# Zero products in TensorE's two first waits, and a level loop rotated by one group

## The chip, the cores and the metric

The kernel runs on one core of a Trainium2 chip. The metric is device time in microseconds (us) for one execution, as the median of several runs.

## The reference

Three stages follow one another for 4 batches of 768 tokens. First a gated linear attention with 8 heads of 48 columns, whose state is decayed and updated at every token:

```
for t in range(S):
    state = alpha[:, :, t, :, None] * state + np.einsum('bhd,bhe->bhde', k[:, :, t], v[:, :, t])
    y[:, :, t] = np.einsum('bhd,bhde->bhe', q[:, :, t], state)
```

Then a block with a low-rank mix over the tokens and a ReLU network of width 1536:

```
h = x.transpose(0, 2, 1) @ U @ V
u = x + h.transpose(0, 2, 1)
x = u + np.maximum(u @ w_ch1, 0.0) @ w_ch2
```

Then a second gated network: a product with `w_in` and a ReLU, a normalised half that is mixed over the tokens by `w_spatial`, a gate and a product with `w_out`. Inputs and output are float32.

## The kernel before

Five engines run programs of their own and meet only at semaphores. TensorE (PE) does all matrix products, VectorE (DVE), ScalarE (ACT) and GpSimd (POOL) the work between them, and SyncE (SP) issues the loads.

The attention of one batch is cut into two groups of four heads. In the text group 0 is the one whose tiles are `K`, `Q`, `AL`, `Qd`, `Ad` and `A`, and group 1 of the first batch the one whose tiles end in `_side`. Within chunks of 128 tokens the scores are built over eight levels, n = 0 to 7: level n pairs blocks of `block_size(n)` tokens. For each of the levels 0 to 5 and each group g the same round is made:

- ACT spreads the queries of the level into `Qd` (`first_spread`, L1080; two copies). It needs PE's products of the level before, since `Qd` is one buffer, and the queries scaled by POOL (`scale_q`, L670).
- PE multiplies them with the keys (`first_level`, which calls `square_scores`, L778): 48 small products of 32 by 32, which the trace records as 96. For group 0 they go to `SB`, for group 1 to `ZB`.
- DVE takes the scores under a mask (`take`, L1397) into `Ad` and scales the keys for the next level (`scale_k`, L1377).

PE's code for this is a hardware loop of six turns over n, with group 0 and group 1 in the turn. Levels 6 and 7 follow in straight code (L826 and L838), then transposed keys (L853), key-value products (L866), outputs (L883, L892) and the token mix (L916). After that PE runs the dense products of the first network (L901, L989 to L991), with the attention of the next batch in between.

At the very start nothing but loads and memsets can run. SP issues queries, decays and keys of group 0 and then of group 1. DVE clears four areas (L1678, L1679, semaphore `zeroed_s`), waits for the decays, and multiplies them up in `first_decay` and `totals` (L1384). PE waits for `zeroed_s`, for the keys (`ld_k`) and for the first spread queries. ACT later copies totals of group 1 into the bank `ZB0` (`total_copies`, L1117).

`w2h` holds weights of the first network, which are loaded and split long after the start. `ZB0` is the first of three banks of PSUM that group 1 and the network share.

Of the kernel before, what the change touches and what calls it, by code (L numbers as in the profile page):

```python
# [7 lines left out]
F32 = mybir.dt.float32  # L8
# [5 lines left out]
P = 128  # L14
# [14 lines left out]
GROUPS = HEADS // (2 * PAIRS)  # L29
# [15 lines left out]
MASKED = 6  # L45
# [141 lines left out]
def vector_slots(slots):  # L187

    out, waiting = [], []
    for j, unit in enumerate(UNITS1):  # L190
        now = []
        for g, n in slots[j]:
            now += waiting
            waiting = [(g, n, piece) for piece in range(vector_pieces(n))]
            now += waiting
            waiting = []
            if n == START_STEP:
                now.append((g, START, 0))
            if n == PREFIX_STEP:
                now.append((g, PREFIX, 0))  # L200
        if not slots[j]:
            now += waiting[:1]
            waiting = waiting[1:]
        out.append(now)
    assert not waiting
    return out


def vector_pieces(n):

    return 2 if n < MASKED else NKV if n == KV_STEP else int(n < LEVELS)
# [14 lines left out]
SPLIT_V = {(0, T_STEP): [0], (1, T_STEP): [1], (1, KV_STEP): [2]}  # L226
IN_PSUM = (3, 4, 5, 2)
SPLITS2 = {2: W1_PIECES + 3, 3: W1_PIECES + 4, 4: W1_PIECES + 5}
VECTOR_SLOTS = [vector_slots(slots) for slots in SLOTS]


def build(nc, q, k, al, v, u_w, v_w, w1, w2, win, wst, wout, bias, ident_d, mask_d, out):
# [3 lines left out]
    with ExitStack() as ctx:  # L236
# [11 lines left out]
        def sem(name):  # L248
            return ctx.enter_context(nc.semaphore(name))
# [6 lines left out]
        V_in, _ = place("V_in", [RANK3, SEQ], o)  # L256
# [13 lines left out]
        early, _ = place("early", [P, STAGE * PIECE], o + 2 * 4 * DB * FF1 + 4 * STAGE * PIECE)  # L270
# [4 lines left out]
        w2h, o = place("w2h", [P, F1B, DM], o, F32R)  # L275
# [54 lines left out]
        x2, _ = place("x2", [P, DB, SEQ], at_xn)  # L330
        x2l, _ = place("x2l", [P, DB, SEQ], at_xn, F32R)
# [5 lines left out]
        winf, _ = place("winf", [P, DB, FF2], o)  # L337
        winl, o = place("winl", [P, DB, FF2], o, F32R)
        BF, _ = place("BF", [P, 7, HS, TH], o)
# [9 lines left out]
        AF, _ = place("AF", [P, 7, HS, HF], o)  # L349
        AL, o = place("AL2", [P, 7, HS, HF], o, F32R)  # L350
        gf, _ = place("gf", [P, FGB, SEQ], o)
        gl, o = place("gl", [P, FGB, SEQ], o, F32R)
        partial, _ = place("partial", [P, FGB, SEQ], o)
# [4 lines left out]
        wof, _ = place("wof", [P, FGB, DM], o)  # L358
# [14 lines left out]
        ZB = [ps(f"ZB{i}") for i in range(DB)]  # L373
# [77 lines left out]
        gl_done = sem("gl_done")  # L451

        passed = sem("passed")
        stored = [sem(f"stored{i}") for i in range(2)]


# [200 lines left out]
        def _(pool):  # L657
# [88 lines left out]
            for b in range(BATCH - 1):  # L746
                for g in range(GROUPS):
                    for n in range(2, LEVELS):
                        scale_q(b + 1, g, n)
                        if b == g == 0 and n - 1 in SPLITS2:  # L750
                            split_low(SPLITS2[n - 1])
                        if g == 0 and b:
# [20 lines left out]
        def _(pe):  # L773
# [9 lines left out]
            def first_level(g, n):  # L783

                w = space(0, g)
                pe.wait_ge(ld_k[g], 16)
                pe.wait_ge(qd_ready[g], 2 * n + 2)

                pe.wait_ge(k_ready[g], n + 1)
                square_scores(level_bank(w, n, True), w.K, w.Qd[0]).then_inc(score_done[g], 1)  # L790
# [185 lines left out]
            def down(b, f):  # L976
# [5 lines left out]
                for d in range(DB):  # L982
# [7 lines left out]
                    nc.tensor.matmul(bank, w2l[:, i, cols], hi, start=False, stop=False)  # L990
                    nc.tensor.matmul(bank, w2h[:, i, cols], lo, start=False, stop=(i == F1B - 1)).then_inc(z_done, 1)  # L991

            def two_group(b, j, first):
                stage, i, h, _, _, at = TWO.groups[j]
                bank = TB[at]
                th = slice(h * TH, (h + 1) * TH)
                last_use, wrapped = TWO.last_use(j)
                if not wrapped:
                    read(pe, TWO, last_use, b)
                elif not first:  # L1000

                    read(pe, TWO, last_use, b - 1)
                else:

                    pe.wait_ge(h_lo, NF * BATCH)
                    if bank in ZB:
                        pe.wait_ge(z_read, NU * (BATCH - 1) + NU - DB + ZB.index(bank) + 1)
                if stage == "v":
                    pe.wait_ge(win_lo, DB)

                    pe.wait_ge(x2_lo, DB * (b + 1))
                    last = split_product(bank[:, 0:FG],
                                         lambda x, d: (x2h, x2l)[x][:, d, i * P:(i + 1) * P],
                                         lambda y, d: (winh, winl)[y][:, d, FG:FF2], [(d, d) for d in range(DB)], DB)
                elif stage == "g":
                    last = split_product(bank[:, 0:TH],
                                         lambda x, d: (winh, winl)[x][:, d, i * P:(i + 1) * P],
                                         lambda y, d: (x2h, x2l)[y][:, d, th], [(d, d) for d in range(DB)], DB)
                elif stage == "s":
                    k = SEVEN.index(i)  # L1020
                    fp = slice(h * P, (h + 1) * P)
                    pe.wait_ge(b_lo, SPLIT_B.index(k) + 1)
                    pe.wait_ge(ah_done, 7 * b + k + 1)
                    for m in range(HS):
                        for y, w in enumerate((BH[k][:, m, :], BL[:, k, m, :])):
                            nc.tensor.matmul(bank[:, 0:TH], AH[:, k, m, fp], w, start=(i in OPENS and m == y == 0),  # L1026
                                             stop=False, skip_group_check=True)
                    pe.wait_ge(al_done, 7 * b + k + 1)
                    for m in range(HS):
                        last = nc.tensor.matmul(bank[:, 0:TH], AL[:, k, m, fp], BH[k][:, m, :],  # L1030
                                                start=False, stop=(m == HS - 1), skip_group_check=True)
                else:
                    pe.wait_ge(wo_lo, 1)
                    rows = slice(i * P, (i + 1) * P)
                    gates = NHALF * FGB * b + (NHALF * FGB if i < HS else 3 * FP)
                    pe.wait_ge(gh_done, gates)
                    for f in range(FGB):
                        for w in (woh, wol):
                            nc.tensor.matmul(bank[:, 0:DM], gh[:, f, rows], w[:, f, :], start=(f == 0 and w is woh),  # L1039
                                             stop=False, skip_group_check=True)  # L1040

                    pe.wait_ge(gl_done, gates)
                    for f in range(FGB):
                        last = nc.tensor.matmul(bank[:, 0:DM], gl[:, f, rows], woh[:, f, :], start=False,
                                                stop=(f == FGB - 1), skip_group_check=True)
                last.then_inc(two_done, 1)

            pe.wait_ge(zeroed_s, 4)
            with pe.Fori(0, MASKED) as n:
                for g in range(GROUPS):  # L1050
                    first_level(g, n)
            for g, n in LAST_STEPS:
                att_step(0, g, n, True)

# [13 lines left out]
            for j in range(TWO.n):  # L1068
                two_group(0, j, True)
# [5 lines left out]
        def _(act):  # L1075
# [35 lines left out]
            def total_copies(g):  # L1111
                w = space(0, g)

                act.wait_ge(tot_ready[g], 4)
                act.wait_ge(zeroed_s, 4)
                for L in (4, 8, 16):
                    nc.scalar.copy(psum_total(w, L), w.tot[L]).then_inc(tot_psum[g], 1)  # L1117

# [196 lines left out]
            for b in range(BATCH - 1):  # L1315
                for j, (kind, i, _) in enumerate(UNITS1):
                    for g, n in SLOTS[b][j]:
                        att_step(b + 1, g, n, False)
                        if b == g == 0 and n in SPLITS2:
                            split_high(SPLITS2[n])  # L1320
                        na, ng = after(b + 1, g)
# [38 lines left out]
        def _(dve):  # L1360
# [83 lines left out]
            def first_level(g):  # L1444

                w = space(0, g)
                dve.wait_ge(ld_mask, 16)
                dve.wait_ge(zeroed_s, 4)
                take(0, g, 0)
                scale_k(0, g, 0)  # L1450
                dve.wait_ge(qd_ready[g], 4)
                dve.wait_ge(tot_ready[g], 1)
                qq = odd(Q[g][:, :], 1).rearrange("p n l -> p (n l)")
                nc.vector.tensor_tensor(qq, qq, w.tot[2], ALU.mult).then_inc(q_ready[g], 1)
# [217 lines left out]
            def aggregate(b, i):  # L1672
                dve.wait_ge(stat_done, NT * b + i + 1)
                dve.sem_inc(passed, 1)
                nc.vector.bn_aggr(mv[:, i, :], stats[:, i, :]).then_inc(mv_done, 1)

            for w in (main_space, side_space):
                nc.vector.memset(w.Ad[:, :, :, :], 0.0).then_inc(zeroed_s, 1)  # L1678
                nc.vector.memset(w.KVB[:, UNITS * BLOCK:512], 0.0).then_inc(zeroed_s, 1)  # L1679
# [32 lines left out]
            for b in range(BATCH):  # L1712
                for j, (kind, i, _) in enumerate(UNITS1):
                    if b < BATCH - 1:
                        for g, n, piece in VECTOR_SLOTS[b][j]:
                            na, ng = after(b + 1, g)
# [60 lines left out]
```

## Time and profile before

| | us |
|---|---|
| median of 3 runs | 728.19 |
| lowest and highest run | 728.19, 728.77 |
| span of the profiled execution, first to last instruction | 723.9 |
| PE busy in that span | 697.6 (96%) |
| DVE, ACT, POOL busy | 394.7, 340.2, 213.5 |

Of the profiled execution the trace gives only the span; the runs are timed around it, so some 4.3 us (728.19 - 723.9) lie outside the span. A busy PE is not a PE at full rate: at its slower clock the same products fill more time.

### The profile page before, as it was taken

How to read it: one execution, taken by the hardware profiler on the slowest of the kernel's cores; microseconds unless marked ns; L12 is line 12 of the kernel's file. 1: busy time of each engine (PE TensorE's matmuls, PEld its weight loads, DVE VectorE, ACT ScalarE, POOL GpSimd, SP SyncE). 2: the span in 40 equal slices, each digit the busy share in tenths (PEclk: the TensorE clock that was granted, in tenths of full speed). 3: DMA queues.
4: the chain of work that ended last, by engine and by line, in shares of the span. 5: the costliest groups of instructions: out<-in, count | busy, mean ns of one | idle time of the engine just before them, and what ended most of it. 6: DMA issues, size and time to landing. Idle time of an engine off the chain costs nothing.

```text
span 723.9 us, 25699 instructions
## 1 busy us (share of the span) xinstructions
PE 697.6 (96%) x11336; PEld 661.9 (91%) x11336; DVE 394.7 (55%) x666; ACT 340.2 (47%) x575; POOL 213.5 (29%) x143
## 2 busy tenths in 40 slices
PE   2799999999999999999999999999999999999998
PEld 2688989899899999999999999999998998999998
DVE  6898766546645644755552415125834842871671
ACT  5987655463654454555453332335523432532422
POOL 6704660410540310350220331461360060043022
PEclk9999999999999999999999999999999999999999
DMA  8415410411301221401100341011110101101001
GB/s 359 170 48 182 150 46 4 152 49 37 122 11 39 86 79 39 156 3 47 36 3 3 116 139 64 32 44 56 65 45 23 66 23 43 65 0 65 0 0 65
DMA packets 16524, 49.48 MB, mean 68 GB/s; under 512 B 1616, under 2 KB 9552, under 8 KB 15920
## 3 DMA queue, kind: packets, MB, share of 16 engines
q1 hardware_dynamic: 16432, 48.09, 19.1%
q8 instruction: 77, 1.26, 0.7%
q14 instruction: 15, 0.12, 0.1%
HBM read 38.65 MB, written 9.44 MB: 66 GB/s over the span
## 4 chain that ended last, share of the span: by engine, by line
PE 90%; DVE 3%; ACT 1%; issue 1%; DVEq 0%
PE HB L901 25%; PE ZB L989 7%; PE ZB L991 7%; PE ZB L990 7%; PE SB L901 6%; PE SB L1026 5%; PE SB L778 4%; PE ZB L901 4%; PE SB L883 2%; PE SB L1030 2%; PE ZB L1039 2%; PE ZB L1026 2%; PE SB L892 2%; PE SB L1039 2%; PE SB L838 1%; DVE K L1377 1%
## 5 line engine op out<-in xcount | busy, mean ns | idle before, releaser
L1557 DVE SCALAR_TENSOR_TENSOR hid_lo<-HB,hid_hi 128x384 fp32r<-128x384 f32 x92 | 51.2, 557 | 138.3 <-ACT hid_hi L1233 137.8
L1233 ACT ACTIVATE hid_hi<-HB 128x384 fp32r<-128x384 f32 x92 | 45.3, 492 | 157.6 <-PE HB L901 157.4
L989 PE MATMUL ZB<-hid_hi,w2h 128*128 128x384 f32 x288 | 98.2, 341 | 0.0
L901 PE MATMUL HB<-uh,w1h 128*128 128x384 f32 x276 | 97.7, 354 | 0.2 <-DVE ul L1553 0.2
L991 PE MATMUL ZB<-hid_lo,w2h 128*128 128x384 f32 x288 | 96.5, 335 | 0.0
L990 PE MATMUL ZB<-hid_hi,w2l 128*128 128x384 f32 x288 | 96.3, 334 | 0.0
L901 PE MATMUL HB<-uh,w1l 128*128 128x384 f32 x276 | 92.5, 335 | 0.2 <-issue 0.2
L901 PE MATMUL HB<-ul,w1h 128*128 128x384 f32 x276 | 92.5, 335 | 0.0
L1080 ACT COPY Qd<-Q 48x768 f32<-48x768 f32 x84 | 73.2, 871 | 14.2 <-POOL Q L670 5.2
L727 POOL TENSOR_TENSOR gl<-gf,gh 128x384 fp32r<-128x384 f32 x32 | 33.6, 1048 | 144.1 <-ACT gh L1273 143.8
L670 POOL TENSOR_TENSOR Q<-Q,bk 112x768 f32<-112x768 f32 x14 | 25.5, 1824 | 162.9 <-ACT Qd L1080 162.9
L778 PEld LDWEIGHTS SB<-Qd,K 112*32 112x32 f32 x4032 | 42.0, 116 | 22.6 <-issue 17.2
L670 POOL TENSOR_TENSOR Q<-Q,small 112x768 f32<-112x768 f32 x26 | 42.7, 1641 | 65.3 <-PE SB L826 31.2
L778 PE MATMUL SB<-Qd,K 112*32 112x32 f32 x4032 | 46.7, 205 | 13.3 <-DMA K<-in_k 9.3
L1377 DVE TENSOR_TENSOR K<-K,small 112x768 f32<-112x768 f32 x26 | 48.8, 1877 | 16.8 <-PE SB L838 9.5
L989 PEld LDWEIGHTS ZB<-hid_hi,w2h 128*128 128x128 f32 x288 | 54.0, 188 | 0.9
L1649 DVE BATCH_NORM_STATS2 stats<-vf 128x6 f32<-128x512 f32 x24 | 16.5, 692 | 69.8 <-ACT vf L1277 69.8
L901 PEld LDWEIGHTS HB<-uh,w1h 128*128 128x128 f32 x276 | 51.7, 187 | 2.9 <-DVE ul L1553 0.3
L990 PEld LDWEIGHTS ZB<-hid_hi,w2l 128*128 128x128 f32 x288 | 54.1, 188 | 0.0
L991 PEld LDWEIGHTS ZB<-hid_lo,w2h 128*128 128x128 f32 x288 | 54.1, 188 | 0.0
L901 PEld LDWEIGHTS HB<-uh,w1l 128*128 128x128 f32 x276 | 51.9, 188 | 0.5 <-issue 0.5
L901 PEld LDWEIGHTS HB<-ul,w1h 128*128 128x128 f32 x276 | 51.8, 188 | 0.0
(269 smaller groups left out, 1519.4 us busy)
## 6 DMA issues: line engine op xcount, KB each, us to landing
Q<-in_q SPq DMA_DIRECT2D x8, 768.0 KB, 5.8
AL<-in_al SPq DMA_DIRECT2D x7, 768.0 KB, 4.6
K<-in_k SPq DMA_DIRECT2D x7, 768.0 KB, 4.4
Vt<-in_v SPq DMA_DIRECT2D x8, 576.0 KB, 3.8
mid<-x2s SPq DMA_DIRECT2D x8, 576.0 KB, 3.5
x<-mid SPq DMA_DIRECT2D x4, 1152.0 KB, 5.2
out<-o_sb SPq DMA_DIRECT2D x24, 192.0 KB, 1.8
x2s<-in_w SPq DMA_DIRECT2D x9, 384.0 KB, 4.3
```

The costliest lines, as they stand in the source:

```text
L670: nc.gpsimd.tensor_tensor(qq, qq, t.broadcast_to([ROWS, FLAT // (2 * L), L]), ALU.mult).then_inc(q_ready[g], 1)
L727: nc.gpsimd.tensor_tensor(gl[:, f, t], gf[:, f, t], gh[:, f, t].bitcast(F32), ALU.subtract).then_inc(gl_done, 1)
L778: last = nc.tensor.matmul(bank[j * BLOCK:(j + 1) * BLOCK, u * BLOCK:(u + 1) * BLOCK], keys[:, first_key:first_key + BLOCK], queries[:, u, ...
L901: last = nc.tensor.matmul(dst, weights(x, w), moving(y, m), start=(n == 0 and x == y == 0), stop=(n == total - 1 and y == 1))
L989: nc.tensor.matmul(bank, w2h[:, i, cols], hi, start=(i == 0), stop=False)
L990: nc.tensor.matmul(bank, w2l[:, i, cols], hi, start=False, stop=False)
L991: nc.tensor.matmul(bank, w2h[:, i, cols], lo, start=False, stop=(i == F1B - 1)).then_inc(z_done, 1)
L1026: nc.tensor.matmul(bank[:, 0:TH], AH[:, k, m, fp], w, start=(i in OPENS and m == y == 0), stop=False, skip_group_check=True)
L1080: nc.scalar.copy(space(a, g).Qd[0 if first else n % 2][r, :, hh, :].rearrange("p u (n l) -> p u n l", l=block_size(n)), targets(Q[g][r, :] ...
L1233: nc.scalar.activation(hid_hi[:, i % HID, :], up_bank(i)[:, 0:TILE], ACT.Relu).then_inc(h_hi, 1)
L1377: nc.vector.tensor_tensor(kk, kk, t.broadcast_to([ROWS, FLAT // (2 * L), L]), ALU.mult).then_inc(k_ready[g], 1)
L1557: nc.vector.scalar_tensor_tensor(hid_lo[:, i % HID, :], up_bank(i)[:, 0:TILE], 0.0, hid_hi[:, i % HID, :].bitcast(F32), ALU.max, ALU.subtr ...
```

## The change

DVE clears three rows of `w2h` (128 partitions by 1152 elements) as its first work and raises `spare_zeroed`. PE waits for that, runs 20 products of 128 by 512 on the zeroes into `ZB0`, then level 0 of group 0, then 14 more of these products, and raises `spare_done`. The loop over the levels is turned by one group: group 0's level 0 stands ahead of it, each of five turns runs group 1 of one level and group 0 of the next, and group 1's level 5 stands behind it. ACT waits for `spare_done` before it copies group 1's totals into `ZB0`. The wait of PE for `zeroed_s` comes behind the first 20 products.

```diff
+SPARE_FRONT, SPARE_BETWEEN = 20, 14
...
+            def spare_products(n):
+
+                for _ in range(n):
+                    last = nc.tensor.matmul(ZB[0][:, :], w2h[:, 0, 0:P], w2h[:, 1:3, 0:256], start=True, stop=True)
+                return last
+
...
+            pe.wait_ge(spare_zeroed, 1)
+            spare_products(SPARE_FRONT)
             pe.wait_ge(zeroed_s, 4)
-            with pe.Fori(0, MASKED) as n:
-                for g in range(GROUPS):
-                    first_level(g, n)
+            first_level(0, 0)
+            spare_products(SPARE_BETWEEN).then_inc(spare_done, 1)
+            with pe.Fori(1, MASKED) as n:
+                first_level(1, n - 1)
+                first_level(0, n)
+            first_level(1, MASKED - 1)
...
                 act.wait_ge(zeroed_s, 4)
+                if g:
+                    act.wait_ge(spare_done, 1)
...
+            nc.vector.memset(w2h[:, 0:3, :].bitcast(F32), 0.0).then_inc(spare_zeroed, 1)
             for w in (main_space, side_space):
```

On PE, at the start of the program, these rows stood before (`SB` and `Qd_76` are group 0, `ZB` and `Qd_side` group 1; the branches and register rows are the loop's):

```order
L1049 UNCONDITIONAL_BRANCH
L787 ISA
L789 REGISTER_ALU
L778 MATMUL SB<-Qd_76,K 32x32 x48
L787 ISA
L789 REGISTER_ALU
L778 MATMUL ZB<-Qd_side,K_side 32x32 x48
L1049 REGISTER_ALU
L1049 COMPARE_AND_BRANCH
L826 MATMUL SB<-Q_69,K 32x32 x48
```

and these stand there now:

```order
L999 MATMUL ZB<-w2h 128x512 x20
L781 MATMUL SB<-Qd_76,K 32x32 x48
L999 MATMUL ZB<-w2h 128x512 x14
L1062 UNCONDITIONAL_BRANCH
L790 ISA
L781 MATMUL ZB<-Qd_side,K_side 32x32 x48
L790 ISA
L792 REGISTER_ALU
L781 MATMUL SB<-Qd_76,K 32x32 x48
L1062 REGISTER_ALU
L1062 COMPARE_AND_BRANCH
L781 MATMUL ZB<-Qd_side,K_side 32x32 x48
```

The two blocks of zero products are new; the sequence of the real products, group 0 and group 1 in turn, is the one of before, and the loop's branch has moved from behind group 1 to behind group 0.

On DVE, from the start of its program, before:

```order
L1678 MEMSET Ad 128x768
L1679 MEMSET SB 128x128
L1678 MEMSET Ad_side 128x768
L1679 MEMSET HB 128x128
L1384 TENSOR_TENSOR bk<-AL 112x768
```

and now:

```order
L1693 MEMSET w2h 128x1152
L1695 MEMSET Ad 128x768
L1696 MEMSET SB 128x128
L1695 MEMSET Ad_side 128x768
L1696 MEMSET HB 128x128
L1400 TENSOR_TENSOR bk<-AL 112x768
```

One memset stands ahead of the four others and of the first product of decays; nothing else on DVE has moved.

## Rows read from the trace of the kernel before

**Rows 1.** The page: busy time, granted clock in 40 slices, the chain by engine
```profile
PE 697.6 (96%) x11336; PEld 661.9 (91%) x11336; DVE 394.7 (55%) x666; ACT 340.2 (47%) x575; POOL 213.5 (29%) x143
...
PEclk9999999999999999999999999999999999999999
...
PE 90%; DVE 3%; ACT 1%; issue 1%; DVEq 0%
```

**Rows 2.** Timeline, 0 to 17 us: start, length, engine, line, operation, tiles, idle before
```profile
0.98 0.70 DVE L1678 MEMSET Ad<- 128x768 f32 x1 [0.98 <-PEq L1770]
...
9.28 1.51 PE L778 MATMUL SB<-Qd,K 112*32 112x32 f32 x96 [9.28 <-DMA K<-in_k]
10.12 0.63 DVE L1384 TENSOR_TENSOR small<-small 112x48 f32<-112x48 f32 x3
...
15.00 1.51 PE L778 MATMUL ZB<-Qd_side,K_side 112*32 112x32 f32 x96 [4.21 <-DMA K_side<-in_k]
...
16.12 0.48 ACT L1117 COPY ZB<-bk_side 112x384 f32<-112x384 f32 x1 [0.72 <-DVE small_side L1384]
```

**Rows 3.** Timeline of PE, 36 to 100 us: the same kinds of products early and late
```profile
36.42 1.50 PE L826 MATMUL SB<-Q,K 48*32 48x32 f32 x96 [0.34 <-DVE K L1377]
...
40.33 2.82 PE L838 MATMUL SB<-Q,K 48*64 48x64 f32 x48
...
67.49 1.03 PE L778 MATMUL SB<-Qd,K 112*32 112x32 f32 x96
...
93.26 1.04 PE L826 MATMUL SB<-Q,K 48*32 48x32 f32 x96 [0.59 <-issue]
...
97.78 1.61 PE L838 MATMUL SB<-Q,K 48*64 48x64 f32 x48
```

**Rows 4.** Stretches: from:to length, PE busy, weight loads, DVE, ACT, POOL, clock, DMA
```profile
16.90:25.00 8.10, 5.99 (x384) 5.46 (x384) 6.99 (x11) 7.86 (x11) 3.55 (x2) 1.00 1.04 377
25.00:36.00 11.00, 8.98 (x576) 8.27 (x576) 9.68 (x13) 9.55 (x12) 9.61 (x7) 1.00 0.12 49
36.40:39.65 3.25, 2.49 (x155) 2.32 (x155) 2.96 (x4) 2.12 (x5) 0.00 (x0) 1.00 0.02 5
39.65:44.60 4.95, 4.95 (x119) 4.89 (x120) 4.21 (x7) 4.79 (x10) 0.00 (x0) 1.00 0.02 5
44.60:48.20 3.60, 3.24 (x42) 2.82 (x39) 3.48 (x7) 3.49 (x8) 0.00 (x0) 1.00 0.02 5
```

**Rows 5.** Groups by shape, PE, 44.75 to 45.7 us: the end of L838
```profile
L838 PE MATMUL ZB<-Q,K_side 48*64 48x64 f32 x19 | 1.1, 291 | 0.0
```

**Rows 6.** What DVE waited for, 7 to 49 us: total, times, longest
```profile
DVE bk L1384 <- DMA AL<-in_al: 4.2, 1, 4.2
DVE Ad L1397 <- PE SB L778: 0.8, 2, 0.4
DVE K_side L1377 <- PE ZB L826: 0.7, 1, 0.7
```

**Rows 7.** Timeline of DVE, 7 to 49 us
```profile
11.07 1.01 DVE L1397 COPY_PREDICATED Ad<-masks,SB 128x384 f32<-128x384 uint32 x1 [0.32 <-PE SB L778]
...
21.76 1.05 DVE L1397 COPY_PREDICATED Ad_side<-masks,ZB 128x384 f32<-128x384 uint32 x1 [0.29 <-DVEq L1491]
23.26 1.06 DVE L1397 COPY_PREDICATED Ad<-masks,SB 128x384 f32<-128x384 uint32 x1 [0.45 <-PE SB L778]
...
37.03 0.95 DVE L1377 TENSOR_TENSOR K_side<-K_side,ZB 112x768 f32<-112x768 f32 x1 [0.19 <-DVE Ad_side L1397]
38.08 0.96 DVE L1377 TENSOR_TENSOR K<-K,small 112x768 f32<-112x768 f32 x1
38.95 0.95 DVE L1433 TENSOR_TENSOR Q<-Q,small 112x768 f32<-112x768 f32 x1
40.56 0.96 DVE L1377 TENSOR_TENSOR K_side<-K_side,small_side 112x768 f32<-112x768 f32 x1 [0.65 <-PE ZB L826]
...
46.62 1.45 DVE L1460 COPY bk<-SB 128x448 f32<-128x448 f32 x3
```

**Rows 8.** The chain that ended last, 30 to 70 us
```profile
39.06 0.58 issue
...
48.21 1.10 PE SB L866 x40
```

**Rows 9.** Timeline of ACT, 9 to 50 us
```profile
29.24 1.69 ACT L1080 COPY Qd_side<-Q 48x768 f32<-48x768 f32 x2 [0.30 <-PE ZB L778]
...
48.40 0.37 ACT L1186 COPY bk_side<-ZB 128x224 f32<-128x224 f32 x1
```

**Rows 10.** Timeline of PE, second network: products of 128 by 512
```profile
487.10 0.39 PE L901 MATMUL SB<-winh,x2h 128*128 128x512 f32 x1
487.33 0.39 PE L901 MATMUL SB<-winh,x2l 128*128 128x512 f32 x1
```

More of the change, by code:

```diff
@@ L453, in build @@
         passed = sem("passed")
+        spare_zeroed = sem("spare_zeroed")
+        spare_done = sem("spare_done")
         stored = [sem(f"stored{i}") for i in range(2)]
```

## The prediction

> **What bounds the kernel now.** The page gives PE 96% of the span and 90% of the chain that ended last [rows 1]. So a gain has to come from a place where PE is slow, or where something holds PE up. The change touches only the first 36 us, so I read the timeline there. PE's first products wait for the keys of group 0 until 9.28 us, and group 1's for theirs until 15.00 [rows 2]. Both are waits for a load. Nothing in the change moves a load, so zero products cannot shorten them; they can only change the state in which PE leaves them.
>
> That state shows when one kind of product is compared early and late. The 96 records of L778 take 1.51 us at 9.28 and at 15.00 [rows 2], and 1.03 us at 67.49; L826 takes 1.50 at 36.42 and 1.04 at 93.26; L838 takes 2.82 at 40.33 and 1.61 at 97.78, which is 1.75 times [rows 3]. So PE ran at the lower of its two clocks (1.2 and 2.4 GHz) from the start. In the last products of L838 the mean record is down from 311 to 291 ns [rows 5], so the rise lies near 45 us. The column of the granted clock says full speed all along [rows 1, 4]; where it and the durations disagree I go by the durations. Before the rise PE was busy 5.99 of 8.10 us, 8.98 of 11.00, 2.49 of 3.25, and then 4.95 of 4.95 us [rows 4].
>
> Next: who sets the pace between 9 and 48 us? DVE does. Its waits there are few: 4.2 us for the decays, which end at 7.1, then 0.8 us in two waits for PE's L778 and 0.7 us for L826 [rows 6]. Everything else on it is work, or the short pause of about 0.19 us between `take` and `scale_k` [rows 7]. At 48.21 PE waits for DVE's last copy of transposed keys and is on the chain from there [rows 8]. So what DVE gains by 48 us the kernel gains, and hardly more.
>
> **The change, step by step.**
>
> *The memset.* 768 columns take 0.70 us [rows 2], so 1152 take 1.05, from 0.98 to 2.03. The four others end 1.05 later, at 4.0, and DVE has nothing to do until 7.1 [rows 6]. Cost nothing; without the 4.2 us of waiting for `AL` it would be 1.05.
>
> *The 20 products ahead.* Dense products of 128 by 512 follow each other every 0.227 us at the full clock (487.10 to 487.33) [rows 10]; 23 such steps in a row, from 486.65 to 491.86, have this mean. At the lower clock no row shows them; the nearest bound is L838's 1.75 times, 0.40 us, and the other bound is the ratio of the two clocks, 0.45. I take 0.43. They start at about 2.2. If the clock rises 5 us later, after as much unbroken work as the 4.95 us of rows 4, it is 7.2; 11.6 products are done, and 8.4 more at 0.227 end at 9.1. That is just ahead of the keys at 9.28, so nothing is lost. If the clock rises only at the end, the block ends at 2.2 + 20 x 0.43 = 10.8.
>
> *Level 0 of group 0* then takes 1.03 in place of 1.51 and ends at 10.31. DVE is done with its totals at 10.75 [rows 2] and can go on at once instead of at 11.07: **-0.29 us**, the wait of 0.32 less a start-up of some 0.03.
>
> *The 14 products between* end at 10.31 + 14 x 0.227 = 13.5, before the keys of group 1 at 15.00. At the lower clock they would take 14 x 0.43 = 6.0. ACT's new wait for them is covered, since it copies into `ZB0` only at 16.12 [rows 2]: 2.6 us of cover. Behind it on ACT stand all further spreads, so past 15.8 each microsecond would delay the levels.
>
> *Levels 1 to 5.* Each group of products is 0.48 shorter. DVE waited for one of them: 0.45 at 23.26. The pause between two takes that its own semaphores force is 0.29, as at 21.76 [rows 7], so only **-0.16 us** comes out. In the levels 3 to 5 DVE never waits for PE, and a PE that is earlier only waits longer. ACT gains its 0.30 at 29.24 [rows 9], which DVE doesn't see.
>
> *Level 6.* DVE finishes `K_side` (from 37.03, so at 37.98) 0.45 earlier, at 37.53. It need not wait for L826 of group 0 (36.0 to 37.0 now) and goes on at 37.63 instead of 38.08. `K` and `Q` take 0.87 and 0.95, until 39.45. L826 of group 1 starts at 37.65 and needs 1.04, and perhaps the 0.58 of issue that stands in its middle [rows 8], so it ends by 39.3. `K_side` starts at 39.45 instead of 40.56: the wait of 0.65 is gone, **-0.66 us**. From there DVE is busy without a pause to its copies of the transposes at 46.62 [rows 7]. L838 at 1.61 needs DVE's queries of 40.3 at the latest and is no obstacle.
>
> *The side path on ACT.* Its copies of `bk_side` end at 48.77 (48.40 + 0.37) [rows 9]; ACT gets about 0.9 of it by an earlier L826, so it ends near 47.9, while L866 of group 1 would start at 48.0. It fits with nothing to spare.
>
> *The loop.* The order of the products is kept, and the branch stands where PE has waited for group 1's queries or keys anyway: nothing.
>
> Sum: 0.29 + 0.16 + 0.66 = 1.1 us. Against the profiled execution that is a span of 723.9 - 1.1 = 722.8; with the 4.3 us outside the span, 727.1, against the median of 728.19. The most that DVE's waits for PE can give is 0.8 + 0.7 = 1.5.
>
> **The rivals.**
>
> *The clock falls again in the levels.* In rows 4 PE was busy 82% between 25 and 36 us and the clock stayed low. With products of 1.03 for 1.51 the same stretch is filled to 56%. No row shows the higher clock kept or lost over such a stretch. If it falls before 23 us, only the first 0.29 remains, and the rise at 45 us stays as it was: 727.9. The Trainium skill, "TensorE: Matmul & The Clock Gate", section "A second HAM failure mode: psum-queue depth-cycling", tells of a kernel in which small pauses of PE between groups of products made the clock swing between its two rates; by that rule this case would be the one to expect, and no run here shows it yet.
>
> *The zero products overrun (slower).* The place is the front block. If the clock rises only at its end, level 0 of group 0 starts at 10.8, ends at 11.8 at the full clock, and DVE's take starts about 1.0 later than the 11.07 of before. Of that the later 0.82 comes back: 728.4. If it doesn't rise until the second block has run, level 0 ends at 12.3, the 14 end at 18.3, and group 1's level 0 at 19.8, where it ended at 16.5 before (15.00 + 1.51): +3.3, 731.5, or 730.7 with what comes back. It decides at a front block that ends after 9.7 us, and at a second one that ends after 15.5.
>
> *More than the profile shows.* The rise near 45 us is that of one execution. In the timed ones it may come later, and then L853 to L883, which PE's pace sets from 48.21 on, would also be slow before. L866 and the first three L883 last some 3.9 us; each us of them at the lower clock costs about 0.4. That would add 0.5 to 1.5 us to the gain: 725.6 to 726.6.
>
> *No effect at all,* because products on zeroes leave the clock low: that is the second form of the overrun, and it costs as there.
>
> **How the numbers follow.** Clock kept, as summed: 0.47 (own range 726.7 to 727.5). Clock lost in the levels: 0.29, near 727.9. Overrun: 0.11, 728.4 to 731.5. More than the profile: 0.13. The runs of before lie 0.6 apart, which widens each. The range 726.1 to 728.6 leaves out most of the overrun and half of the last case. A measurement of this kernel can tell 0.2%, 1.46 us, from no change. Faster by more than that: all of the last case and a quarter of the first, 0.25. Slower by more: the worse part of the overrun, 0.08, and 0.02 for what I don't see. The same: 0.65.
>
> **What would show it.** In the new trace the 96 records of L781 should take 1.03 us in every level; if some take 1.5, the first rival is right from there on. The front block should start near 2.2, show a step from some 0.43 to 0.227 between starts, and end before 9.3; PE's waits for both loads should end at about 9.3 and 15.0. The DVE row at 23.26 should begin near 22.8, that of 40.56 near 39.4, and L869 (the old L866) near 47.1. ACT's wait for `spare_done` should not appear. The prediction is wrong if ACT or POOL becomes the one that DVE waits for in the levels, or if the new straight code makes PE wait for issue longer than the 0.58 of rows 8.

## The result, and the profile after

The changed kernel has a median of 732.23 us (729.28 to 739.5, 11 runs), the kernel before one of 727.24 us (725.56 to 728.77, 11 runs, the three of the table above among them). The ratio is 1.0082 with a 95% interval of 1.0056 to 1.0107: slower by 5 us, where 1.1 us of gain was forecast and 728.6 was the upper end of the range. The ratio is estimated from all the runs; it is not the quotient of the two medians, which is 1.0069. The profiled execution has a span of 731.0 us against 723.9. That is 7.1 us more, for the execution profiled before was a quick one: in every run of that kernel whose span is known the time lies 2.1 to 2.3 us above the span, not the 4.3 that stand under "Time and profile before", so a span of 723.9 belongs to some 726.1 us. In the changed kernel 1.8 us lie outside (732.83 - 731.0).

The clock first. The stretches of the changed kernel, PE alone; the columns are from:to, length, PE busy and its records, granted clock, share and rate of the DMA:

```profile
2.14:5.80 3.66, 3.66 (x9) 1.00 0.94 358
5.80:8.65 2.85, 2.85 (x13) 1.00 1.01 408
8.65:16.00 7.35, 4.42 (x110) 1.00 1.01 416
16.00:50.00 34.00, 26.37 (x1350) 0.50 0.33 120
50.00:53.50 3.50, 3.50 (x32) 0.50 0.02 5
53.50:60.00 6.50, 6.50 (x244) 0.99 0.35 124
```

Nine zero products in 3.66 us are 0.41 us each; from 5.8 us on they are fast. At 16.0, after 2.5 us in which PE had nothing to do, the clock falls to half (1.2 GHz) and stays there until 53.5; before, L838 sped up near 45 [rows 5]. The products on PE's timeline say the same, and more:

```profile
2.14 6.51 PE L999 MATMUL ZB<-w2h 128*128 128x512 f32 x20 [2.14 <-DVE w2h L1693]
9.16 1.02 PE L781 MATMUL SB<-Qd,K 112*32 112x32 f32 x96 [0.51 <-issue]
10.11 3.47 PE L999 MATMUL ZB<-w2h 128*128 128x512 f32 x14
16.09 1.51 PE L781 MATMUL ZB<-Qd_side,K_side 112*32 112x32 f32 x96 [2.52 <-DMA K_side<-in_k]
...
37.63 0.97 PE L829 MATMUL SB<-Q,K 48*32 48x32 f32 x55
39.62 0.79 PE L829 MATMUL SB<-Q,K 48*32 48x32 f32 x41 [1.02 <-issue]
40.37 1.39 PE L829 MATMUL ZB<-Q,K_side 48*32 48x32 f32 x86
43.22 0.42 PE L829 MATMUL ZB<-Q,K_side 48*32 48x32 f32 x10 [1.46 <-issue]
43.56 2.82 PE L841 MATMUL SB<-Q,K 48*64 48x64 f32 x48
...
52.87 1.40 PE L869 MATMUL SB<-Vt,bk 128*48 128x48 f32 x40
```

The front block ends at 8.65 and costs nothing. Level 0 of group 0 takes 1.02 us, every later one 1.51 as before. Two things stand here that the prediction did not have. The keys of group 1 land at 16.09 instead of 15.00 [rows 2]. And L829, the old L826, is cut twice by a pause for issue, 1.02 and 1.46 us, where before there was one of 0.58 and a start-up of 0.16. What DVE waited for, 7 to 53 us, shows who is now ahead of it:

```profile
DVE Ad_side L1413 <- PE ZB L781: 2.1, 4, 1.1
DVE K_side L1393 <- PE ZB L829: 1.4, 1, 1.4
DVE K L1393 <- PE SB L829: 1.1, 1, 1.1
DVE Ad L1413 <- PE SB L781: 0.4, 1, 0.4
DVE K_side L1393 <- PE ZB L841: 0.2, 1, 0.2
```

That is 5.2 us of waits for PE in place of 1.5 [rows 6]. L869 starts at 52.87 against 48.21 [rows 8].

The rest comes later, on PE again, in the first batch of the network. Its timeline from 78 to 90 us has these two rows with a wait, where before there was one of 0.50 for issue at 88.29:

```profile
82.51 0.95 PE L781 MATMUL SB<-Qd,K 112*32 112x32 f32 x87 [1.31 <-issue]
88.37 1.02 PE L781 MATMUL SB<-Qd,K 112*32 112x32 f32 x96 [1.58 <-ACT Qd L1094]
```

The token mix of the four batches starts at 60.38, 177.19, 290.96 and 404.40 us before, and at 65.34, 185.15, 298.71 and 411.50 in the changed kernel. So it is 4.96 us late at the first, 7.96 at the second, 7.1 at the last: two thirds are lost before 65 us, 3.0 us between 65 and 185, and nothing after. Between the first two token mixes the pauses of PE above 0.1 us add up to 5.1 us in place of 2.5, which is most of the 3.0.

### The profile page after: what moved, and what is told of

Read it like the earlier page. It is cut to its first block, busy times and chain, and to the rows that moved or that the text cites. A ratio compares the mean times of both kernels' runs of the same rounds, so it can differ in the third digit from the quotient of the medians.

```text
span 731.0 us, 25764 instructions
## 1 busy us (share of the span) xinstructions
PE 709.1 (97%) x11370; PEld 671.4 (92%) x11370; DVE 398.2 (54%) x667; ACT 339.9 (47%) x575; POOL 213.0 (29%) x143
## 3 DMA queue, kind: packets, MB, share of 16 engines
q8 instruction: 79, 1.29, 0.7%
## 4 chain that ended last, share of the span: by engine, by line
PE 91%; DVE 2%; issue 1%; ACT 1%; DVEq 0%
PE HB L904 25%; PE ZB L992 7%; PE ZB L994 7%; PE ZB L993 7%; PE SB L904 6%; PE SB L1035 5%; PE SB L781 4%; PE ZB L904 4%; PE SB L886 2%; PE SB L1039 2%; PE ZB L1048 2%; PE ZB L1035 2%; PE SB L895 2%; PE SB L841 2%; PE SB L1048 2%
## 5 line engine op out<-in xcount | busy, mean ns | idle before, releaser
L1249 ACT ACTIVATE hid_hi<-HB 128x384 fp32r<-128x384 f32 x92 | 45.3, 492 | 161.6 <-PE HB L904 161.4
L1413 DVE COPY_PREDICATED Ad<-masks,SB 128x384 f32<-128x384 uint32 x42 | 33.9, 806 | 34.5 <-PE SB L781 30.1
```

Of the source, the lines that this page charges most:

```text
L1249: nc.scalar.activation(hid_hi[:, i % HID, :], up_bank(i)[:, 0:TILE], ACT.Relu).then_inc(h_hi, 1)
L1413: nc.vector.copy_predicated(dst, m, src).then_inc(a_dve[g], 1)
```

## The experiments

Two theories were set against each other. **Theory F**: the loss is in the code. PE's instructions come from memory in blocks. The page of the changed kernel counts 79 packets and 1.29 MB for the queue `q8 instruction`, 16 KB each, and one such packet falls between 13 and 14 us, before group 1's keys land; before the change the first in the loads' time fell between 18 and 19. Where many small products stand in straight code PE can come to the end of a block before the next is there, and each block end that is moved falls into other work. The Trainium skill, "Runtime: NRT & Kernel Launch", section "Instruction fetch mechanics", says that the sequencer fetches 16 KiB blocks of 256 instructions by its own DMA queue, and that a crossing is mostly hidden; the size agrees with 1.29 MB in 79 packets, "mostly hidden" does not hold for the pauses above. **Theory C**: the loss is in the zero products and the clock. Each ratio below is to the kernel before, run on the same chip, with its 95% interval, and not the quotient of the medians.

**One part alone.** `rotation_only` has the rotated loop and nothing else:

```diff
-            pe.wait_ge(spare_zeroed, 1)
-            spare_products(SPARE_FRONT)
-            spare_products(SPARE_BETWEEN).then_inc(spare_done, 1)
-                if g:
-                    act.wait_ge(spare_done, 1)
-            nc.vector.memset(w2h[:, 0:3, :].bitcast(F32), 0.0).then_inc(spare_zeroed, 1)
```

> Only the loop is rotated; no zero products, no memset, no new wait of ScalarE. Theory F (issue: TensorE runs out of instructions where small products stand in straight code, and all later code has moved): the time rises by the pauses for issue, some 0.2 us in L829 and some us between 60 and 177 us, together 1 to 4 us over before. Theory C (clock: the loss is all in the clock, which fell in the second wait and rose late): TensorE is at the lower clock from the start and rises near 45 us as before, so the time is that of before within 0.5 us. Theory K (the keys of group 1 land later because of the change): they land at 15.0 as before.

737.77 us, ratio 1.0103 (1.005 to 1.0156, four runs): rotation alone loses as much as the whole change, and it never raises the clock early (it rises at 52.5, before at 45.3). The keys land at 14.99. The profiled execution is the slowest of the four, 741.2 us. Its timeline shows two long pauses of PE, one in the midst of group 0's level 1 while the loads run, another before a level of the next batch, and a row of DVE that belongs to the second:

```profile
16.30 0.63 PE L781 MATMUL SB<-Qd,K 112*32 112x32 f32 x27
20.98 1.18 PE L781 MATMUL SB<-Qd,K 112*32 112x32 f32 x69 [4.05 <-issue]
...
95.55 5.96 DVE L1388 TENSOR_TENSOR K<-K,small 112x768 f32<-112x768 f32 x1
101.61 1.51 PE L781 MATMUL SB<-Qd,K 112*32 112x32 f32 x96 [4.90 <-issue]
```

The first pause stands between two products of one group, so it can't be a wait for data. The second is put down to issue too, but it need not be one: PE goes on 0.1 us after DVE has scaled the keys `K` that this level multiplies, and that one instruction took 5.96 us, where it takes 0.96 at the start [rows 7] and at most 3.23 in the network of the kernel before. POOL worked from 95.50 to 100.69 us beside it, almost without a gap. So a pause of PE may also be paid a second time, by work of DVE that then falls beside POOL's; no run was made to show this. The 96 records after the second pause take 1.51 us, and the clock stays at half from 100.3 to 107.1, so a long pause costs the clock as well. Theory F is right in kind, and its 1 to 4 us were too few. `front_only` has the memset and the front block, and the loop as before:

```diff
-            first_level(0, 0)
-            spare_products(SPARE_BETWEEN).then_inc(spare_done, 1)
-            with pe.Fori(1, MASKED) as n:
-                first_level(1, n - 1)
-                first_level(0, n)
-            first_level(1, MASKED - 1)
+            with pe.Fori(0, MASKED) as n:
+                for g in range(GROUPS):
+                    first_level(g, n)
```

> The memset and the 20 zero products ahead, the loop as before. Theory C: the clock rises near 6 us and falls again within the wait for group 1's keys; the rise that counts comes near 45 us or later, and each us that it is later than 45.3 costs about 0.4 us. Theory F: the code moves by only some 44 instructions, and group 1's level 5 stays in the loop, so the pauses in L829 stay near 0.7 us and the time is within 1 us of before. Theory K: the keys land at 15.0 if the second block of products was what delayed them, at 16.1 if the memset or the first block was.

732.88 us, ratio 1.0066 (1.004 to 1.0092). Group 1's level 0 starts at 16.66. Theory F's "within 1 us of before" failed: some 40 instructions (20 products and their loads of weights) are not few. So the code was moved with no other change. `pad44` is the kernel before with

```diff
+            for _ in range(44):
+                pe.sem_inc(passed, 1)
             pe.wait_ge(zeroed_s, 4)
             with pe.Fori(0, MASKED) as n:
```

> The kernel before with 44 empty semaphore instructions on TensorE at its start, in the wait for the first keys: as many instructions as the front block of zero products has, and nothing else. Theory F (instruction blocks): the next block of TensorE's instructions is fetched near 13.5 us instead of 18.0, in the midst of the first loads, and group 1's keys land 1 to 1.6 us later than the 15.0 of before; a long pause for issue appears in L826 of group 1 (near 1.2 us); the time rises by 2 to 5 us. Theory C (clock, or the zero products themselves, are what costs): nothing happens, the time is within 0.5 us of before.

735.07 us, ratio 1.0132 (1.0099 to 1.0164). This is the test that settles the kind of cause: no product, no memset and no rotation, nothing waits for that semaphore, and the last of the 44 is done at 7.5 us, before the first keys; yet at least as much is lost as by the whole change. Its PE timeline has the late keys and the longer pause in L826, as expected, and a pause of 2.09 us in the dense products of the network, after which they take 0.52 us instead of 0.34 until the clock is back at 96.0:

```profile
16.28 1.51 PE L778 MATMUL ZB<-Qd_side,K_side 112*32 112x32 f32 x96 [5.08 <-DMA K_side<-in_k]
...
39.06 0.71 PE L826 MATMUL ZB<-Q,K_side 48*32 48x32 f32 x35 [0.18 <-issue]
40.98 1.07 PE L826 MATMUL ZB<-Q,K_side 48*32 48x32 f32 x61 [1.21 <-issue]
...
88.16 0.34 PE L990 MATMUL ZB<-hid_hi,w2l 128*128 128x384 f32 x1
90.59 0.48 PE L991 MATMUL ZB<-hid_lo,w2h 128*128 128x384 f32 x1 [2.09 <-issue]
90.86 0.52 PE L989 MATMUL ZB<-hid_hi,w2h 128*128 128x384 f32 x1
```

Between the first two token mixes it takes 123.07 us in place of 116.81. The pauses of PE above 0.1 us add up to 5.8 us there in place of 2.5, and the 6.8 us at the lower clock (89.2 to 96.0) cost at most half of that, 3.4 us by an estimate from the two rates. So the clock has a part in the loss, but behind a pause and not by the zero products.

**The same work in less code.** `front_loop` and `loops` are `front_only` and the changed kernel with the products in a hardware loop:

```diff
-                for _ in range(n):
-                    last = nc.tensor.matmul(...)
-                return last
+                with pe.Fori(0, n // 5):
+                    for _ in range(5):
+                        one()
+                return one()
```

> The memset and 21 zero products ahead, but in a hardware loop of four turns of five, so that they take some 20 instructions of code; the level loop as before, no products between. Theory F: the keys of group 1 land at 15.0 again unless the block boundary is passed before, the pauses are as in the kernel before, and the time is at least 3 us below that of front_only (732.9) and within 1 us of before. Theory C: it is that of front_only within 1 us, as TensorE does the same work at the same times.

728.22 us, ratio 1.0023 (1.0009 to 1.0037), against 1.0066 of `front_only` with the same work. The keys land at 14.86, the clock rises near 6.7 and falls near 13.5 us, and all levels from group 1's first are slow. It misses "within 1 us of before" (726.47 on that chip) by 0.75 us. The clock is back for good at 44.2 us, and the first token mix starts at 60.43, in the kernel before at 60.38.

> The changed kernel with both blocks of zero products in hardware loops (21 and 11 products); the level loop rotated, so 384 small-product instructions stand in straight code. Theory F: the instruction block that holds the end of the loop's turn is asked for only when group 1's level 0 starts, so the keys land at 15.0, but group 0's level 1 is cut by a pause for issue of about 4 us, as in rotation_only; the time is above the changed kernel's median by 0 to 5 us. Theory C: as the changed kernel within 1 us.

732.29 us, ratio 1.0099 (1.0075 to 1.0122). Theory C's "as the changed kernel" holds in microseconds, but not beside rotation_only, which has no products and a like ratio. Theory F's long pause at group 0's level 1 did not come; L829 and L841 have pauses of 1.63 and 0.86 us. Group 1's level 0 starts at 15.20.

**The same code without the work.** `tiny` is the changed kernel, `tiny20` is `front_only`, each with

```diff
-                    last = nc.tensor.matmul(ZB[0][:, :], w2h[:, 0, 0:P], w2h[:, 1:3, 0:256], start=True, stop=True)
+                    last = nc.tensor.matmul(ZB[0][0:BLOCK, 0:BLOCK], w2h[0:BLOCK, 0, 0:BLOCK], w2h[0:BLOCK, 1, 0:BLOCK], start=True, stop=True)
```

> The changed kernel with each zero product of 128 by 512 replaced by one of 32 by 32: the same number of instructions in the same places, but almost no work. Theory F (instruction blocks): the loss is all in the code, so the time is that of the changed kernel or a little more, 4 to 9 us above before; the stretch from the first token mix to the second takes about 119.8 us as in the changed kernel, against 116.8 before. Theory C (the dense products or the clock cost the time): it falls back to that of before within 1 us. TensorE should stay at the lower clock until 45 us or later.

734.44 us, ratio 1.0112 (1.0066 to 1.0159).

> Memset and 20 products of 32 by 32 ahead, level loop not rotated: the code of front_only without its work. Theory F: as front_only (732.9) or slower, group 1's keys land at 16 to 16.7 us. Theory C: as before within 1 us.

733.15 us, ratio 1.0069 (1.0047 to 1.0091), against 1.0066 with dense products. Both bear out theory F, and theory C falls: without the work the loss is as large. `tiny20` is the cleaner of the two, for its clock does what it did before (it rises at 46.1 us, before at 45.3). In `tiny` it was to stay low until 45 us, but it rose at 31.5, fell at 38.3, rose at 48.6, fell at 58.8 behind a pause of 2.51 us in L886, and was back at 62.2. A number of theory F missed as well: between the token mixes `tiny` takes 116.7 us (67.90 to 184.59), not 119.8. With the code in the same place a pause may come in one execution and not in another; the runs of `tiny` lie between 732.4 and 743.3 us.

**The second block longer.** `between25` has 25 products in place of 14, `between25_again` is the same kernel once more, `tiny25` its twin with products of 32 by 32:

```diff
-SPARE_FRONT, SPARE_BETWEEN = 20, 14
+SPARE_FRONT, SPARE_BETWEEN = 20, 25
```

> 25 zero products in place of 14 in the second wait; they end near 15.8 us at the higher clock. Theory C1 (the idle TensorE of 2.5 us dropped the clock): it stays up through the levels, the 96 records of L781 take 1.03 us, and the time falls by 2 to 4 us against the changed kernel. Theory C2 (the small products of the levels don't hold it): it falls anyway a few us later, before 25 us, and the time stays within 1 us of the changed kernel. Theory F: no change of the pauses but for 22 more instructions.

729.46 us, ratio 1.0023 (1.0003 to 1.0043). In its stretches (columns as in [rows 4]) the clock stays up through the wait and the first levels, falls near 27.8, comes back near 31 and falls again near 38, under the same small products:

```profile
16.00:27.00 11.00, 6.33 (x578) 5.55 (x576) 9.04 (x12) 10.20 (x15) 4.82 (x3) 1.00 0.99 361
27.00:31.00 4.00, 2.82 (x192) 2.71 (x192) 3.00 (x4) 3.42 (x5) 3.77 (x3) 0.59 0.04 14
31.00:38.00 7.00, 3.86 (x348) 3.37 (x339) 6.24 (x9) 5.44 (x7) 4.63 (x3) 0.99 0.01 2
```

It looked like a gain of 3 us by the clock.

> The kernel with 20 and 25 dense zero products once more, beside its twin with small ones on the same chip. Both theories: 0.0 to 0.5% above before, as in the first run of it.

729.26 us, ratio 1.0021 (1.0007 to 1.0035). In this execution of the same kernel the clock fell at 21.6 already and stayed low until 52.3.

> The same code as between25, with every zero product made 32 by 32. What it lies above between25 is what the dense products and the clock give, at an unchanged place of all code. Theory F with the small gain forecast for the clock: 0.8 to 2 us above between25. If it is 4 us or more above, the clock is worth more than the waits of VectorE for TensorE, which were read as its upper bound; if it is the same, the gain of between25 over the changed kernel came from the 22 instructions by which its code is moved.

729.67 us, ratio 1.0024 (1.0006 to 1.0043): the twin at the lower clock until 53 us is as fast, and the 0.8 to 2 us that theory F gave the clock were too many. The early clock is worth 0.4 us by the medians, less than the intervals tell; how long it was held differs from one execution to the next. What made `between25` faster than the changed kernel, and `tiny25` faster than `tiny` (734.44), are the 22 instructions by which the code is moved. They do not act before the first token mix, which starts at 65.34 in `tiny25` as in the changed kernel, but behind it: the second comes 115.4 us later, not 119.8.

**The place of the code.** `padded` is the changed kernel with 60 empty semaphore instructions behind the second block, to bring later code back to its old place within a block:

```diff
             spare_products(SPARE_BETWEEN).then_inc(spare_done, 1)
+            for _ in range(60):
+                pe.sem_inc(passed, 1)
```

> The changed kernel with 60 empty semaphore instructions on TensorE in the wait for group 1's keys, so that all code from level 1 on stands, modulo 256 instructions, where it stood before. Theory F: the pauses for issue between 60 and 177 us go back to those of before, which gives back 2 to 3 us of the 3.0 by which this stretch grew; the pauses in L829 stay near 2 us. Theory C: nothing changes against the changed kernel but what the clock does.

735.4 us, ratio 1.0097 (1.0067 to 1.0128). Between the token mixes it takes 116.7 us (70.94 to 187.60), as foretold, but `tiny` does so without padding, so this proves nothing. And an empty semaphore instruction is not free: they stand 0.15 us apart in the trace, 9 us for 60, and delay group 1's level 0 to 19.96. A pause for issue of 3.99 us in group 0's level 1 follows, at 26.74. The next three move the code by small products instead, 0.055 us each, with the loop not rotated and the front block in place of `SPARE_FRONT = 20` set to 100, 128 and 109, that is by 200, 256 and 218 instructions:

```diff
-SPARE_FRONT, SPARE_BETWEEN = 20, 14
+SPARE_FRONT, SPARE_BETWEEN = 128, 14
```

> Memset and 100 products of 32 by 32 ahead, level loop not rotated: all later code moved by 204 instructions, nearly the position that it has in the changed kernel (452, or 196 modulo 256), but without a rotated loop. Theory F: the stretch from the first token mix to the second takes about 119.8 us as in the changed kernel; up to the first token mix the pauses for issue are shorter than in the changed kernel, since group 1's level 5 stays in the loop. Theory C: nothing changes against before.

731.67 us, ratio 1.0057 (1.003 to 1.0084). The 119.8 us were missed again (117.1). The shorter pauses up to the token mix came in L829 only (0.90 us against 2.48); another of 1.33 us stands in L886.

> Level loop not rotated, 128 products of 32 by 32 ahead: all later code moved by 256 instructions, a whole block. If the place within a block decides the pauses (theory F, place), all pauses from L826 on are where they were before, and the time is within 0.3% of before, the rest being a later landing of group 1's keys. If the number of instructions that is moved matters, or chance does, it is 3 us or more above, as the other moved kernels.

728.38 us, ratio 1.0018 (1.0006 to 1.003), as theory F with the place foretold, though its keys land late too. The pause in L829 cuts the same product as before, behind 57 records, where 20 products ahead put it behind 37. The rows are, two by two, the kernel before, `tiny20` and `tinypad256`:

```profile
38.09 0.98 PE L826 MATMUL ZB<-Q,K_side 48*32 48x32 f32 x57 [0.16 <-issue]
39.65 0.76 PE L826 MATMUL ZB<-Q,K_side 48*32 48x32 f32 x39 [0.58 <-issue]
...
39.55 0.75 PE L829 MATMUL ZB<-Q,K_side 48*32 48x32 f32 x37 [0.19 <-issue]
41.36 1.06 PE L829 MATMUL ZB<-Q,K_side 48*32 48x32 f32 x59 [1.06 <-issue]
...
39.87 0.97 PE L829 MATMUL ZB<-Q,K_side 48*32 48x32 f32 x57 [0.17 <-issue]
41.95 0.76 PE L829 MATMUL ZB<-Q,K_side 48*32 48x32 f32 x39 [1.10 <-issue]
```

Its length is not that of before, 1.10 us for 0.58, and a new pause of 1.22 us cuts level 0 of group 0.

> Level loop not rotated, 109 products of 32 by 32 ahead: moved by about 218 instructions, the place within a block that tiny25 and between25 have, without their rotated loop. Theory F, place: at most the 0.24% of tiny25 above before, and less by the 1 to 2 us of pauses in L829 that the straight level 5 costs. If it is far above tiny25, place within a block is not what made tiny25 faster than tiny.

728.13 us, ratio 1.0007 (0.9994 to 1.002): no difference from before that can be told, with 218 instructions more than it.

The place of the pause can be counted. A small product stands as one record and takes two instructions, itself and the load of its weights. In group 1's L826 or L829 the pause comes behind 57 records before; behind 37 with 20 products ahead (`tiny20`, `front_only`), 35 with 44 empty instructions (`pad44`), 50 in `front_loop`, 57 in `tinypad256`, 85 in `tinypad200` (57 - 100 + 128) and 76 in `tinypad218` (57 - 109 + 128). The two pauses of the changed kernel, behind 55 records of group 0 and 86 of group 1, lie 127 records or 254 instructions apart. So these pauses stand at the ends of blocks of 256 instructions, which theory F had assumed.

| instructions moved, less whole blocks | kernel | ratio |
|---|---|---|
| 0 | `tinypad256` | 1.0018 |
| 0, with 9 us of empty instructions | `padded` | 1.0097 |
| 14 | `front_loop` | 1.0023 |
| 40 | `front_only`, `tiny20` | 1.0066, 1.0069 |
| 44 | `pad44` | 1.0132 |
| 128 | `rotation_only` | 1.0103 |
| some 160 | `loops` | 1.0099 |
| 196 | changed kernel, `tiny` | 1.0082, 1.0112 |
| 200 | `tinypad200` | 1.0057 |
| 218 | `tinypad218` | 1.0007 |
| 218, loop rotated | `between25` twice, `tiny25` | 1.0023, 1.0021, 1.0024 |

## Why the prediction was wrong

*The step that failed* is "The loop. The order of the products is kept, and the branch stands where PE has waited for group 1's queries or keys anyway: nothing." The order of the work was costed and the code was not. All of PE's later instructions move by some 452: 68 for the zero products, 384 for two groups of real ones that left the loop for straight code (192 records, each with a load of weights). Moving code with almost no work costs 0.7% at 40 instructions (`tiny20`) and 1.3% at 44 (`pad44`), and nothing that can be told at 218. The same holds for "so nothing is lost" behind the 20 products: their time was covered, their 40 instructions were not. The last sentence of the prediction named a pause for issue longer than 0.58 as what would make it wrong, but gave it neither a price nor a chance, though 0.58 us in L826 stood in the rows. That was the rival to write down: the slower one that I wrote, an overrun of the zero products, had nothing to do with it.

*A second number was taken as fixed.* "Nothing in the change moves a load" is true of the issues, but group 1's keys landed at 16.09 instead of 15.00. They were late in twelve of the kernels here, all but the one before, `rotation_only`, `front_loop` and `loops`, and the traces show by what.

The load raises its semaphore in 16 parts. In these twelve, with or without dense products, 15 parts are in by 15.0 us and the sixteenth at 15.8 to 16.45; in the other four all 16 are in by 14.95. In nine of the twelve an instruction block of 16 KB was fetched at 13.5 to 14.0 us, in the three `tinypad` kernels at 9.6 to 9.8, and from there on one part of each load is late (in `tinypad256` by 1.26 us at 12.1 already); before the block none is by more than 0.3 us. In the kernel before the block comes at 18.0, behind the keys. So the block seems to hold up one sixteenth of each load behind it. `loops` fetches its block at 13.94 and has its keys in at 14.95, and only the sixteenth part of the next load is 0.8 us behind; `tiny25`, with the same 13.94, has late keys: what decides at that edge stays open. Late keys alone cost little: `tinypad218` has them at 16.05 and no loss that can be told (at most 0.20%, 1.5 us).

*The size of each part*, in the profiled execution: the keys 1.1 us, the pauses in L829 1.7 (1.02 + 1.46 for 0.16 + 0.58), L841 to L856 at the lower clock that before had risen near 45 some 1.4 (the lag grows from 3.23 us at L841 to 4.66 at L869), the stretch to the second token mix 3.0. They overlap with each other and with the 0.25 us that was gained. Most of the 3.0 is two pauses: PE is stopped for issue within a level (1.31 us at 82.51) and then waits 1.58 us at the next level for ACT's spread of the queries. The same pair stands in `pad44` (0.85 and 1.49 us) and `rotation_only` (1.42 and 1.54); where no pause above 0.7 us falls into that level, as in `tiny25` and the `tinypad` kernels, the second one is missing too.

*The memset*: right; it ends near 2.1 and DVE still waits 3.0 us for the decays.

*The 20 products ahead*: right. 0.41 us each at the lower clock (0.43 assumed), the clock up at 5.8 (7.2), the end at 8.65 (9.1). The rival of an overrun did not come.

*Level 0 of group 0*: right. DVE's take starts at 10.82 instead of 11.07, 0.25 gained for 0.29.

*The 14 products between*: they ended at 13.6 as forecast, but 2.5 us of idle PE followed and the clock fell at 16.0. The first rival, a fall before 23 us, is what happened, though not as it said: the clock fell behind an idle stretch. `between25` shows that without it the small products hold the clock for a while and not throughout. The Trainium skill, "TensorE: Matmul & The Clock Gate", section "A second HAM failure mode: psum-queue depth-cycling", tells of small pauses that make the clock swing; the trace of `between25` agrees (down at 27.8, up at 31.2, down at 38.0).

*Levels 1 to 6*: the gains of 0.16 and 0.66 did not come at the lower clock. That the clock is worth little, since DVE sets the pace (1.1 us, 1.5 at most), is borne out by `between25_again` and `tiny25`: 0.4 us apart by the medians, though the profiled execution of the first held the clock only to 21.6 us.

Shown is that the loss comes from the place of PE's code and not from its work: `pad44`, `tiny` and `tiny20` lose as much with no dense product. Shown is that a whole block of 256, or 218, gives nearly all of it back. Not shown is what the rotated loop costs by itself: `tiny25` and `tinypad218` stand at about the same place with and without it, 1.0024 and 1.0007, and the intervals overlap. How a pause comes about is seen in part: in the changed kernel, `pad44` and `tiny`, nine pauses for issue of 0.85 to 2.51 us between 38 and 91 us end 2.2 to 2.7 us after the packet of a block starts on its queue, so the pause is what of that time PE has no instructions for. The pauses of some 0.6 us that every kernel has (134.17 before) follow no packet so closely and stay unexplained. In `rotation_only` the packet starts at 18.49, 1.6 us after PE had stopped at 16.93; why it was asked for so late stays open. Open too is how much of the loss at the costly places is this, and how much the waits for ACT and the long scalings on DVE that follow; the same code in two executions does not pause alike. No version here is faster than the kernel before.

## What to carry to other kernels

In this kernel each edit of TensorE's straight code moved the pauses of all that followed, product by product, and cost between nothing and 1.3%. So read the waits for issue, and run a twin that has the same code with almost no work before you credit or blame the work. Try the same edit at a few places of the code before you judge it: filler in a hardware loop took the front block from 1.0066 to 1.0023, but both blocks in loops (`loops`, 1.0099) were no better than straight, and 218 instructions of straight filler cost nothing. A pause that the profile calls issue may be another engine's: look for an instruction that ends just before it. Before warming a clock, ask which engine sets the pace in the stretch: here it was VectorE, whose waits for TensorE were 1.5 us in all.

## What was not expected of the hardware

- 44 instructions that do nothing cost 1.32% (1.0099 to 1.0164); 128 small products (256 instructions) ahead of the same loop cost 0.18%.
- A pause for issue can last 4.05 us (`rotation_only`), and behind 2.09 us of it in dense products the next ones took 0.52 instead of 0.34 us for 5 us (`pad44`).
- An instruction block fetched amid the loads is followed by loads of which one part in 16 lands some 0.8 to 1.9 us after the others; before it none is late by more than 0.3 us.
- One scaling of keys on VectorE (112 by 768) took 5.96 us while GpSimd ran three instructions, and 0.96 in the levels at the start.
- The column of the granted clock reads 1.00 until the first change of the clock that the trace holds, even where products run at the lower rate: 0.41 us each from 2.14 to 5.80 us in the changed kernel.
- An empty semaphore instruction takes TensorE 0.15 us, a product of 32 by 32 with its load of weights 0.055 us at the lower clock (109 in 5.99 us).
